# The fourth turn of the probabilities moves behind the first hard swish in VectorE's order

## What is computed

```python
def _attn_ref(q, kv, w_sr):
    kv_pool = kv.reshape(B, H // r, r, W // r, r, C).mean(axis=(2, 4))
    k = v = kv_pool.reshape(B, -1, C) @ w_sr
    s = scale * (q @ k.transpose(0, 2, 1))
    s = s - s.max(-1, keepdims=True)
    a = np.exp(s)
    a /= a.sum(-1, keepdims=True) + 1e-09
    return a @ v
def _moe_ref(x, w_in, w_out):              # first network, d_ff = 2048
    h = x @ w_in
    g = h * (1.0 / (1.0 + np.exp(-1.702 * h)))
    return g @ w_out
def _moe2_ref(x, w_in, w_out):             # second network, d_ff = 2048
    h = x @ w_in
    return (h * np.clip(h + 3.0, 0.0, 6.0) / 6.0) @ w_out
```

## Time and profile before

| | |
|---|---|
| median of 3 runs | 1339.53 us (1339.42 to 1341.97) |
| profiled execution, its own time | 1341.93 us |
| its span (first to last instruction) | 1340.2 us |
| mean granted clock of TensorE | 0.998 |
| busy TensorE / VectorE / ScalarE | 96% / 78% / 77% |
| instructions TensorE / VectorE / ScalarE | 5748 matmuls / 1073 / 1211 |

### The profile page before, as it was taken

How to read it: one execution, slowest core, us unless ns; L and a number is a source line. 1 busy time by engine, 2 the same in 40 slices (tenths; PEclk the granted TensorE clock), 3 DMA queues, 4 the chain that set the end, 5 groups by cost and what they waited for, 6 DMA issues and landing times.

```text
span 1340.2 us, 18302 instructions
## 1 busy us (share of the span) xinstructions
PE 1283.9 (96%) x5748; PEld 1061.7 (79%) x5748; DVE 1042.5 (78%) x1073; ACT 1034.7 (77%) x1211; POOL 36.2 (3%) x43
## 2 busy tenths in 40 slices
PE   6789999999999999999999999999999999999996
PEld 6578887887887878878878788788788887887775
DVE  4778788788787887787878887888778788887666
ACT  2678778788787787887877878878778778787665
POOL 1900000000000000000000000000000000000000
PEclk9999999999999999999999999999999999999999
DMA  8332203213023032131230321311303203112000
GB/s 267 90 68 50 64 8 71 47 24 71 20 51 70 0 71 47 23 71 26 44 71 0 71 50 21 71 32 38 71 5 65 58 12 71 39 24 64 8 0 17
DMA packets 186948, 65.94 MB, mean 49 GB/s; under 512 B 108720, under 2 KB 179504, under 8 KB 186672
## 3 DMA queue, kind: packets, MB, share of 16 engines
q1 hardware_dynamic: 186928, 65.69, 21.8%
HBM read 23.13 MB, written 6.34 MB: 22 GB/s over the span
## 4 chain that ended last, share of the span: by engine, by line
PE 83%; DVE 8%; ACT 5%; issue 2%; DMA 1%; ACTq 0%; DVEq 0%; SPq 0%
PE pair L784 13%; PE pair L786 13%; PE pair L785 13%; PE bank_av L784 8%; PE bank_av L785 8%; PE bank_av L786 8%; PE bank_out L784 7%; PE bank_out L786 6%; PE bank_out L785 6%; DVE mid_lo L662 3%; DVE work L655 2%; ACT mid_hi L459 2%; ACT work L446 2%; DVE p_turned L613 2%; PE pair L798 1%
## 5 line engine op out<-in xcount | busy, mean ns | idle before, releaser
L662 DVE TENSOR_TENSOR mid_lo<-work,mid_hi 128x1024 fp32r<-128x1024 f32 (+1 forms) x193 | 235.2, 1219 | 137.8 <-ACT mid_hi L459 137.6
L784 PE MATMUL pair<-x_hi,w_hi 128*128 128x512 f32 x768 | 302.6, 394 | 6.6 <-DVE x_lo L638 5.5
L785 PE MATMUL pair<-x_lo,w_hi 128*128 128x512 f32 x768 | 299.9, 391 | 0.0
L786 PE MATMUL pair<-x_hi,w_lo 128*128 128x512 f32 x768 | 299.5, 390 | 0.0
L646 DVE TENSOR_TENSOR mid_lo<-work,mid_hi 128x1024 fp32r<-128x1024 f32 x192 | 237.5, 1237 | 54.0 <-ACT mid_hi L438 54.0
L431 ACT ACTIVATE work<-pair 128x1024 f32<-128x1024 f32 x192 | 197.1, 1027 | 106.5 <-PE pair L786 106.3
L459 ACT ACTIVATE mid_hi<-work 128x1024 fp32r<-128x1024 f32 (+1 forms) x193 | 202.2, 1048 | 48.0 <-DVE work L655 47.0
L655 DVE SCALAR_TENSOR_TENSOR work<-work,pair 128x1024 f32<-128x1024 f32 (+1 forms) x193 | 232.5, 1205 | 8.4 <-ACT work L446 8.3
L446 ACT ACTIVATE work<-pair,half 128x1024 f32<-128x1024 f32 (+1 forms) x193 | 211.9, 1098 | 11.0 <-PE pair L786 10.4
L438 ACT ACTIVATE mid_hi<-work 128x1024 fp32r<-128x1024 f32 x192 | 201.8, 1051 | 4.9 <-PE bank_av L786 3.4
L784 PEld LDWEIGHTS pair<-x_hi,w_hi 128*128 128x128 f32 x768 | 144.5, 188 | 44.8 <-DVE x_lo L638 6.4
(11 more groups left out here) (87 smaller groups left out, 1507.7 us busy)
## 6 DMA issues: line engine op xcount, KB each, us to landing
p_keys<-p_turned SPq DMA_DIRECT2D x368, 96.0 KB, 2.2
inv_b<-inv_dram SPq DMA_DIRECT2D x24, 256.0 KB, 3.3
q_raw<-in_q_dram SPq DMA_DIRECT2D x92, 64.0 KB, 2.0
out_dram<-y_sb SPq DMA_DIRECT2D x92, 64.0 KB, 2.4
kv_sb<-in_kv_dram SPq DMA_DIRECT2D x7, 768.0 KB, 11.1
w_raw<-in_moe_w_in_dram SPq DMA_DIRECT2D x2, 1024.0 KB, 8.2
inv_dram<-inv_t SPq DMA_DIRECT2D x96, 0.5 KB
kv_sb<-in_kv_dram SPq DMA_DIRECT2D x3, 256.0 KB, 11.6
```

What stands on the lines that cost most here:

```text
L662: dve.tensor_tensor(mid_lo[mid2(t, p)][:, part], act2[p % 2][:, part], mid_hi[mid2(t, p)][:, part], ALU.subtract).then_inc(mid2_ready, 1)
L784: pe.matmul(dst, a_hi, b_hi, start=start, stop=False)
L785: pe.matmul(dst, a_hi, b_lo, start=False, stop=False)
L786: return pe.matmul(dst, a_lo, b_hi, start=False, stop=stop)
```

## The change

VectorE's iteration of the kernel has the fourth turn of the next tile's probabilities, `turn_p(i + 1, 3)`, at the end of pair 0, behind act1_lo(i, 0). After the change it stands in pair 1, behind `hard_swish(i - 1, 0)` and ahead of `act2_lo(i - 1, 0)`. No instruction is added or removed, and the programs of the other engines are the same. It bears on the iterations with probabilities to turn, 1 to 22.

```diff
                 for p in range(PAIRS):
                     if p > 0:
                         hard_swish(i - 1, p - 1)
+                    if p == 1 and with_p:
+                        turn_p(i + 1, 3)
                     if p == 0 and with_y:
                         turn_y(i - 2)
...
                     if p == PAIRS - 1:
                         act2_lo(i - 1, p - 1)
-                    if p == 0 and with_p:
-                        turn_p(i + 1, 3)
```

## The result

| | kernel before | changed kernel |
|---|---|---|
| median, first comparison | 1340.34 us (4 runs) | 1322.20 us (4 runs, 1321.35 to 1323.01) |
| ratio, first comparison | | 0.9863, 95% interval 0.9846 to 0.9880 |
| median, second comparison | 1339.47 us (7 runs) | 1321.31 us (4 runs, 1318.64 to 1322.34) |
| ratio, second comparison | | 0.9857, 95% interval 0.9836 to 0.9878 |
| profiled execution, time / span | 1341.93 / 1340.2 us | 1322.82 / 1321.1 us |

The kernel became 1.4% faster, 18.1 us by the medians. The forecast was 19.6 us (1319.9 us, range 1317.0 to 1323.0), and 1322.20 us lies near the upper end of the range. The spans of the two profiled executions differ by 19.1 us, which is 22 times 0.87.

What follows compares the result with a forecast made beforehand. TensorE, 96% busy, was taken to stall each iteration for act2_lo, delayed by the turn ahead of the hard swish. 22 x 0.89 = 19.6 us off the 1339.53 us median, other terms zero, gave 1319.9 us, range 1317.0 to 1323.0.

Steps and rivals of the forecast that it cites:

- rival 2: VectorE's gate wait on the register instruction costs up to 0.10 us more per iteration: 17.4 us gain, 1322.1 us; chance 6%.
- The shift: Without the turn ahead, the hard swish and act2_lo start 0.89 us earlier, and TensorE's projection too, in 22 iterations.
- What remains of the stall: TensorE's projection behind act2_lo still starts 0.23 us late, since the chain from gate to act2_lo is still last.
- The upper bound: TensorE's first matmul behind the stall loses its extra 0.11 us: 1.00 us gain per iteration, 1317.5 us; chance 2%.
- The new place: Behind the hard swish the turn fits VectorE's 1.13 us idle time before act2_lo, leaving 0.29 us.
- Rival 1: The turn holds VectorE longer in its new place and delays act2_lo: 2.9 us gain, 1336.6 us; chance 2%.
- Part 2: Turn behind the hard swish fills VectorE's hole before act2_lo; without cover, each us beyond delays TensorE by as much.
- The wait on the register instruction: VectorE's gate wait before the hard swish, 0.12 us, ends at 628.53, under 628.58 when VectorE is free: cost zero.
- The DMAs: SyncE's shuffles of p_turned land 1.13 us later, still 3.8 us before ScalarE reads them: cost zero.
- Rival 5: Shuffles land after ScalarE wants them, holding the gelus; at 5.2 us later, 0.5 us per iteration, 1350.5 us; chance 2%.
- The rule on repeating gaps: TensorE's repeating stall could mean too few buffers, so moving the turn gives nothing, 1339.5 us; forecast held data late instead.
- rival 4: TensorE's stall stays or turns up at the next projection, so no gain: 1339.5 us; chance 4%.

Runs made afterwards that it cites:

- The fifth experiment: Kernel before, turn still ahead of the hard swish, with project2 of pair 0 finished behind job 5 instead of job 4 in TensorE's order: 1321.30 us, ratio 0.9861.

## Why the prediction was right

- **The time** was 2.3 us above the forecast. 0.8 us of it is the kernel before, with a median of 1340.34 us here where the forecast started from 1339.53; 1.5 us is the gain, 18.1 us in place of 19.6. The measured time is as good as that of rival 2 (1322.1 us), but that agreement is chance: rival 2 has the hard swish start later, and it starts 1.15 us after act1_lo as forecast, with 0.88 us less from stall to stall and not 0.79. That 1322.20 us still lies in the range is owed to a bound that was set for rival 2 and for scatter.
- **The stall and its cause** held: 22 pieces of waiting went, the wait for `mid_lo` fell to 4.6 us (5 to 7 forecast), `p_turned` left the chain. The kernels have between nothing and three turns at the old place; the gap of TensorE was 0.49, 0.96, 1.35, 2.21 and 3.08 us for 0, 1/2, 1, 2 and 3 turns.
- **The shift** was 0.87 us and not 0.89. The missing 0.02 us lies between hard swish and copy: 621.05 - 619.81 = 1.24 us, where the forecast carried over 1.22 us from the earlier trace rows. A hard swish that follows a turn is shown with 1.18 us, one that follows act1_lo with 1.21. Iteration 23 had shown 0.86 us and was the better source, since its hard swish follows act1_lo directly, as in the changed kernel; the copy there starts 1.24 us after it too. By it the sum is 18.9 us, by the place itself 19.6, by the spans 19.1.
- **What remains of the stall** was forecast as 0.23 us, with the restart unchanged. It was 0.25 us with a first matmul of 0.50 us. The upper bound (a free restart) did not come.
- **The new place** of the turn cost nothing: act2_lo waited 0.24 us for the copy (0.29 forecast). Rival 1 did not come, and with two turns there the missing cover showed as Part 2 said.
- **The wait on the register instruction** cost nothing, as forecast, and rival 2 did not come. Its size, 0.12 us by the forecast, stays open: from the gate's end to the hard swish are 0.18 us, but 0.16 to 0.17 us are there too where no register instruction waits for the gate. Only a later gate or a shorter act1_lo would show it.
- **The DMAs** had 3.9 us of slack (3.8 forecast). Rival 5 did not come.
- **The rule on repeating gaps** of the Trainium skill (Perfetto Trace Analysis, Identifying Performance Opportunities), too few buffers, would have given no gain. The gap shrank with no buffer added, by the order alone.
- **No wait took its place**, rival 4. The fifth experiment shows when it would have: once the first stall is hidden otherwise, the second project2 waits for the same late chain.

## What to carry to other kernels

When one engine waits at the same point of every iteration, follow the data back and look in the queue of each engine of the chain for work that nobody needs yet; move it into a hole of that engine inside or behind the chain. Its price at the old place is the distance between starts and not its duration, and the size of the hole bounds what can be put there. Afterwards look at the gaps between starts and not only at the list of waits: the 0.25 us and the slow restart that were left stood in no list and were worth 8.5 to 9 us here, to be had by letting the waiting engine do another job first.

## What the runs showed of the hardware

The longer gaps of TensorE cost more than their length. With 1.31 to 1.37 us from start to start its clock never fell behind one of the 22; with 2.21 us it fell to the lower level, 1.2 GHz, a granted clock of 0.50, behind 6 of 22 gaps, at a price of 1.6 us each; with 3.08 us it did so behind 11 of 22, and 10 of 21 distances were lengthened, by 1.4 to 2.9 us. The Trainium skill (TensorE: Matmul & The Clock Gate, Part 1: The HAM clock gate) says that idleness brings the clock down and activity brings it back, with which these rows agree.

A short gap has a price behind it too: the first 128x512 matmul is shown 0.50 us long in place of 0.39, and the next one starts 0.34 us after it in place of 0.23, also where the gap is only 0.48 us from start to start (623.42, then 623.76).

In a full queue of VectorE the next instruction starts before the shown duration is over: 0.89 us behind the start of a transpose of 0.97 us, 0.49 us behind one of 0.57 us, 1.15 us behind a subtraction of 1.23 us.
